# Batch transposes by DMA, a second buffer for values, a third chunk over two PSUM pairs and a new engine order in a sparse-attention and MLP kernel

## The reference

```python
scores = scale * np.matmul(q, k.transpose(0, 1, 3, 2))
mask_local = (rel >= 0) & (rel < stride)            # stride = 32, heads 0 to 3
mask_strided = (rel >= 0) & (pos[None, :] % stride == pos[:, None] % stride)   # heads 4 to 7
attn = softmax(where(mask, scores, -1e9)) ; attn_out = attn @ v
x = attn_out.transpose(0, 2, 1, 3).reshape(B * S, H * D)      # 4608 x 512
h = x @ w_in                                                  # 512 -> 2048
P = a[0] + a[1] * h + a[2] * h**2 + a[3] * h**3
Q = 1.0 + abs(b[0]) * abs(h) + abs(b[1]) * h**2
out = (P / (Q + 1e-6)) @ w_out                                # 2048 -> 512
```

## Time and profile before

| | us |
|---|---|
| median of 13 runs | 410.68 |
| lowest and highest of them | 408.20, 414.85 |
| the profiled execution | 408.66 |
| its span, first to last instruction | 406.5 |
| DVE busy | 328.6 |
| PE busy | 330.7 |
| ACT busy | 269.7 |

### The profile page before, as it was taken

One profiled execution on the slowest core, in us unless ns is written; L12 is line 12 of the kernel. 1 busy time (PEld: TensorE's weight loads), 2 busy tenths in 40 slices (PEclk: granted clock), 3 DMA queues, 4 the chain that ended last, 5 costly groups with the idle time before them and its releaser, 6 DMA issues.

```text
span 406.5 us, 9652 instructions
## 1 busy us (share of the span) xinstructions
PE 330.7 (81%) x4312; PEld 167.9 (41%) x4352; DVE 328.6 (81%) x279; ACT 269.7 (66%) x236; POOL 154.6 (38%) x203
## 2 busy tenths in 40 slices
PE   2499659988896998789998999997899889688530
PEld 2455334454453555335454544443344445343210
DVE  3539998999841148999999998899899799999930
ACT  3438938794864457985996896399279669685310
POOL 1968735935974992397074009300000000000000
PEclk9759958999999999969999999999699999999955
DMA  8999899879999997596295139443002201222002
GB/s 264 189 162 123 111 200 93 89 90 109 155 158 120 101 166 75 110 92 57 41 108 91 30 79 96 65 79 73 0 0 53 52 19 34 52 53 52 0 21 83
DMA packets 100121, 36.04 MB, mean 89 GB/s; under 512 B 71792, under 2 KB 95024, under 8 KB 100080
## 3 DMA queue, kind: packets, MB, share of 16 engines
q0 software_dynamic: 72800, 16.86, 46.7%
q1 hardware_dynamic: 27280, 18.57, 20.6%
HBM read 36.90 MB, written 9.44 MB: 114 GB/s over the span
## 4 chain that ended last, share of the span: by engine, by line
DVE 40%; PE 39%; ACT 8%; issue 6%; SPq 2%; DMA 2%; DVEq 0%
PE psH L578 16%; PE psO L578 13%; DVE UU L957 6%; DVE T L987 5%; DVE T L981 5%; DVE UU L954 4%; PE psS L578 4%; DVE T L977 4%; DVE T L942 3%; DVE T L984 3%; DVE T L974 3%; PE psA L578 3%; DVE T L979 3%; DVE XR L838 2%; ACT HB L928 2%
## 5 line engine op out<-in xcount | busy, mean ns | idle before, releaser
L578 PE MATMUL psO<-Wout,T 128*128 128x512 bf16 x473 | 113.9, 383 | 11.5 <-issue 3.7
L578 PE MATMUL psH<-XT,Win 128*128 128x512 bf16 x448 | 113.6, 398 | 9.4 <-ACT HB L928 8.9
L928 ACT ACTIVATE HB<-psH 128x1024 bf16<-128x1024 f32 x64 | 65.3, 1020 | 56.3 <-PE psH L578 56.1
L966 ACT ACTIVATE UU<-UU,cst 128x2048 bf16<-128x2048 bf16 (+1 forms) x38 | 72.5, 1909 | 11.9 <-DVE UU L957 11.9
L578 PEld LDWEIGHTS psO<-Wout,T 128*128 128x128 bf16 x512 | 47.5, 99 | 64.1 <-ACT OS L1051 4.8
L969 ACT ACTIVATE UU<-UU 128x2048 bf16<-128x2048 bf16 (+1 forms) x38 | 69.2, 1821 | 0.4
L578 PEld LDWEIGHTS psH<-XT,Win 128*128 128x128 bf16 x448 | 42.4, 99 | 65.1 <-ACT HB L928 12.2
L472 POOL DMA_DIRECT2D VL<-in_v_dram x28 | 24.5, 888 | 62.4 <-PE psA L578 62.0
L987 DVE TENSOR_TENSOR T<-T,UU 128x4096 bf16<-128x4096 bf16 (+2 forms) x23 | 41.6, 1824 | 3.2 <-ACT UU L969 2.8
L957 DVE TENSOR_TENSOR UU<-UU,T 128x4096 bf16<-128x4096 bf16 (+2 forms) x23 | 41.6, 1822 | 0.3
L977 DVE TENSOR_TENSOR T<-T,HB 128x8192 bf16<-128x8192 bf16 (+3 forms) x17 | 41.1, 2416 | 0.5
(11 more groups left out here) (137 smaller groups left out, 391.0 us busy)
## 6 DMA issues: line engine op xcount, KB each, us to landing
out_dram<-OS SPq DMA_DIRECT2D x72, 128.0 KB
kn<-in_k_dram POOLq DMA_DIRECT2D x14, 256.0 KB, 5.6
qn<-in_q_dram POOLq DMA_DIRECT2D x14, 256.0 KB, 6.1
Win<-in_moe_w_in_dram POOLq DMA_DIRECT2D x4, 512.0 KB, 9.8
Wout<-in_moe_w_out_dram POOLq DMA_DIRECT2D x1, 2048.0 KB, 15.6
VL<-in_v_dram POOLq DMA_DIRECT2D x28, 72.0 KB, 3.5
VT<-in_v_dram POOLq DMA_DIRECT2D x56, 32.0 KB, 2.9
VL<-VL SPq DMA_DIRECT2D x7, 153.0 KB, 3.1
```

Of the source, the lines that this page charges most:

```text
L578: return lambda e: e.matmul(out_ap, l, r, start=start, stop=stop, skip_group_check=True)
L928: o2 = add("ACT", (lambda a, hb=hb, ps=ps, f=f: a.activation(hb[:, f:f + 2, :], ps[:, :, :], AF.Copy)), [o1, old], ca(1024), key - 30)
L966: ln = add("ACT", (lambda a, u=u, zl=zl: a.activation(u[:, zl, :], u[:, zl, :], AF.Ln, bias=cst[:, 0:1], scale=1.0)), [d3, cons], 0.28 + w ...
```

## The change

- The strided heads' q and k of batches 1 to 7 are transposed by four DMA transposes per batch, issued by SP (step T), in place of R1 and the copy by DVE. Batch 0 keeps R1. `sT` has a new layout (head ahead of pair).
- The leftover rows of q and k of all batches are transposed by two DMA transposes per batch (step TL), in place of the 24 products and the copy to `LT` by ACT; a small copy by ACT into `kL` remains. The rows lie in `qm` and `km` in runs of 64 for that.
- The second batch's values get a buffer of their own inside `T3[2]`, idle until chunk 2 (`vi`); batch 2 then follows batch 0 in the ordinary buffer. The staging of batch 0's q and k moves to `HB[1]`.
- Chunk 2's steps alternate between pairs H and O as well (`NHO = 3`), and `dense2(c)` follows `dense1(c + 2)` in the program's order.
- `Wout` is loaded after R3 of batch 1; the values of batch 1 are issued ahead of the second half of `Win`; the identity is the first load of all.
- 70 matmuls of 128 columns on the identity (`fill`) depend on its load alone, have the highest keys and stand ahead of the last PE transpose of batch 0's attention.
- Nearly all keys come from a table by kind and by batch or chunk (`KT`, `Key`), so that the order on every engine is a new one.

```diff
+KT = {
+    "L": [-72.4, -237.8, -370.7, 323.1, 600.5, -236.5, -196.6, 245.0],
+    "S": [-680.0, 36.9, -286.2, -371.8, 156.5, 311.6, 229.2, 619.8],
+    "A": [-410.3, -115.4, 44.6, 115.1, -153.3, 41.1, -16.3, 133.2],
+    "AL": [-397.0, 199.6],
...
+    "XT": [-221.2, -555.1, -446.7, 242.3, -29.5, 235.2, 198.6, 337.0],
+    "HB": [95.1, 57.3, -165.0, -358.4, 31.9, -341.6, 222.2, 540.1, 102.5],
...
+class Key:
...
+    def of(self, kind):
+        return Key(kind, self.i, self.off)
+
+    def value(self):
+        return KT[self.kind][self.i] + self.off
...
-    SB, AB, MB, HL = 1.7, 0.0, 2.9, 4
+    HL, NHO, DA, TB, NF0 = 4, 3, 0, 1, 70
...
+    LT = A("LT", [128, 2, 4, 128], BF)
+    NV = 2
+
+    def vi(b):
+        return 1 if b == 1 else 0
...
+    VT = [A("VT0", [128, 4, 4, VS], BF)]
+    VW = [A("VW0", [128, 2, VS], BF)]
+    t3f = T3[2].rearrange("x f c -> x (f c)")
+    VL.append(t3f[:, 0:36 * VS].rearrange("x (m h d) -> x m h d", m=9, h=4))
+    VT.append(t3f[:, 36 * VS:52 * VS].rearrange("x (h g d) -> x h g d", h=4, g=4))
+    VW.append(t3f[:, 52 * VS:54 * VS].rearrange("x (j d) -> x j d", j=2))
...
-    c_idn = cload("c_idn", IDN, np.eye(128), -990)
+    c_idn = cload("c_idn", IDN, np.eye(128), -1005)
...
-    def load_wout(key):
+    def load_wout(key, dep):
         add("POOL", (lambda e: e.dma_start(Wout[:, :, :], w_out.rearrange("(f p) o -> p f o", p=128))),
-            [v_free[0]], 1.3, key, g2, 12.5)
+            dep, 1.3, key, g2, 12.5)
...
-    f32q = T3[2].rearrange("x f c -> x (f c)").bitcast(F32)
+    f32q = HB[1].rearrange("x f c -> x (f c)").bitcast(F32)
...
-        t3_free[2] = [ops]
+        hb_free[1] = [ops]
...
             load_v(1, -940, 0)
-            load_win(2, -930)
-            load_win(3, -929)
-            load_v(1, -920, 1)
+            load_v(1, -930, 1)
+            load_win(2, -920)
+            load_win(3, -919)
             for x in (1, 0):
                 load_qk(1, -909, 2, x)
             load_v(1, -908, 2)
-            load_wout(-890)
         else:
-            key = (b - 2.3) * P
+            key = Key("L", b)
+            if b == 2:
+                load_wout(key + 0.9, [n_free[0][1][0]])
...
+    fill = [add("PE", (lambda e: e.matmul(PS["H"][:, 1, 0:128], IDN[:, :], IDN[:, :], start=True, stop=True,
+                                          skip_group_check=True)), [c_idn], 0.1, 9000.0 + z) for z in range(NF0)]
...
-        base = (b - SB) * P if b > 1 else -100.0 if b else -300.0
+        base = Key("S", b)
...
-        order = ["R1", "R2", "R3", "S", "L", "X"]
+            sets.update(X="A")
+        order = ["T" if b >= TB else "R1", "R2", "R3", "S", "L", "TL", "X"]
         if first:
-            order = ["RL", "X"] if late else ["R1", "R2", "R3", "S", "L"]
+            order = ["TL", "X"] if late else ["T" if b >= TB else "R1", "R2", "R3", "S", "L"]
...
+            if name == "T":
+                tr = []
+                for x, T in ((1, K), (0, Q)):
+                    g = ch_t[x].group()
+                    for y in range(2):
+                        add("SP", (lambda e, x=x, T=T, y=y: e.dma_start_transpose(
+                            sT[:, x, 2 * y:2 * y + 2, :, :].rearrange("x h e p -> x (h e) p"),
+                            T[:, 4 + 2 * y:6 + 2 * y, :].rearrange("x h c -> x (h c)"))),
+                            [n_ev[x, 0, b], t_free["sT"]], 1.25, key.of("ST"), g, 0.6)
+                    n_free[x][0][i] = g.ops
+                    tr.append(g.ops)
+                evs["sT"] = tr
+            elif name == "TL":
+                g = ch_t[2].group()
+                for x, t in ((0, qm[i]), (1, km[i])):
+                    n_free[x][2][i] = g.ops
+                    add("SP", (lambda e, x=x, t=t: e.dma_start_transpose(LT[:, x, :, :], t[:, :])),
+                        [n_ev[x, 2, b], t_free["LT"]], 1.25, key.of("ST"), g, 0.6)
+                evs["LT"] = g.ops
+                evs["kLl"] = add("ACT", (lambda a: a.activation(
+                    kL[:, :, 544:608].rearrange("x a (p g) -> x g a p", g=4),
+                    LT[:, 1, :, 0:32].rearrange("x g (a p) -> x g a p", a=2), AF.Copy)),
+                    [g.ops, t_free["kLl"]], ca(128), key.of("XE" if first and name in ("TL", "X") else "SE"))
...
                 evs["kL"] = [e, ini[id(kL)]]
-            elif name in ("R3", "RL"):
...
-                    deps.append(n_ev[0, 1, b])
-                left = name == "RL" or not first
-                if left:
...
         v_free[iv] = avs
+        if iv == 1:
+            t3_free[2] = avs
...
-                pn = "HO"[npair[0] % 2] if c < 2 else "H"
+                pn = "HO"[npair[0] % 2] if c < NHO else "H"
...
-        if step >= 2:
-            dense2(step - 2, res[step - 2])
+        if step >= 3:
+            dense2(step - 3, res[step - 3])
```

More of the change, by code:

```diff
@@ L412, in bass_strided_sparse_attn__then__act_rational_pade_kernel @@
     ch_s = [chan(f"c_s{i}") for i in range(NV)]
+    ch_t = [chan(f"c_t{x}") for x in range(3)]
     ch_x = [chan(f"c_x{i}") for i in range(NX)]
@@ L650, in scores @@
                                              K[:, 2 * a + hh, 64 * g:64 * g + 64], IDN[:, :], True, True))
-                o1 = add("PE", makers, [n_ev[1, 1, b], c_idn, fr], 0.5 if b else 1.0, key)
+                o1 = add("PE", makers, [n_ev[1, 1, b], c_idn, fr], 1.0, key)
                 n_free[1][1][i] = [o1]
-                e = evac("ACT", kL[:, :, 32:544], ps[:, :, :], [o1, t_free["kL"]], key - 5, 1024)
+                e = evac("ACT", kL[:, :, 32:544], ps[:, :, :], [o1, t_free["kL"]], key.of("XE" if first and name in ("TL", "X") else "SE"), 1024)
@@ new lines, in scores @@
+                for a in range(2):
+                    for g in range(4):
+                        o = (a * 4 + g) * 128
+                        for hh in range(2):
+                            makers.append(tp(pb[64 * hh:64 * hh + 64, 0, o:o + 128],
+                                             Q[:, 2 * a + hh, 64 * g:64 * g + 64], IDN[:, :]))
+                o1 = add("PE", makers, [c_idn, fr, n_ev[0, 1, b]], 0.65, key)
+                n_free[0][1][i] = [o1]
+                e = evac("ACT" if b else "DVE", qL[:, :, :, :].rearrange("x a g p -> x (a g p)"), pb[:, 0, :],
+                         [o1, t_free["qL"]], key.of("XE" if first and name in ("TL", "X") else "SE"), 1024, True)
@@ L726, in scores @@
                                         "x g (r c) -> x c g r", c=2), False, False))
[L727 removed]
+                o1 = add("PE", makers, [evs["kL"], evs["qL"], c_mk, c_idn, fr], 0.85 if b else 1.5, key)
                 e = add("ACT", (lambda a, ps=ps: a.activation(EL[es][:, :, :], ps[:, :, :], AF.Exp, scale=0.125)),
[L729 removed]
+                        [o1, E_free[es]], ca(1024), key.of("XE" if first and name in ("TL", "X") else "SE"))
                 p_free[pn] = [e]
@@ L767, in scores @@
                     ps[:, :, 64:256].rearrange("x j (u i) -> x j u i", i=16), AF.Exp, scale=0.125)),
-                    [o1, E_free[es], ini[id(EW[es])]], ca(384), key - 5)
+                    [o1, E_free[es], ini[id(EW[es])]], ca(384), key.of("XE" if first and name in ("TL", "X") else "SE"))
                 p_free[pn] = [e1, e2]
@@ L856, in attend @@
                 ot = add("PE", [tp(pt[:, 128 * n_:128 * n_ + 128], x[:, 128 * n_:128 * n_ + 128], IDN[:, :])
-                                for n_ in range(4)], [o3, fr_, c_idn], 0.5 if b == 0 else 0.25, key + 0.4)
-                ev = evac("DVE" if T % 2 == 0 else "ACT", dst, pt.rearrange("x (n c) -> x n c", n=4), [ot, wait], key - 20, 512, True)
+                                for n_ in range(4)], [o3, fr_, c_idn, fill if b == 0 and T == 3 else []], 0.5 if b == 0 else 0.25, key + 0.4)
+                ev = evac("DVE" if T % 2 == 0 else "ACT", dst, pt.rearrange("x (n c) -> x n c", n=4), [ot, wait], key.of("N" if key.kind == "A" else "NL"), 512, True)
                 x_prev = fr_
@@ L889, in dense1 @@
     def dense1(c):
[L890 removed]
+        base = Key("M1", c)
         res = []
@@ L1058, in bass_strided_sparse_attn__then__act_rational_pade_kernel @@
     res = {}
-    for step in range(NCH + 2):
+    for step in range(NCH + 3):
         if step < B:
```

154 lines of the change are left out of this document (61 added, 93 removed), and 13 rows, old and new, of the table KT.

## The result

The changed kernel takes 404.61 us (median of 11 runs, 403.07 to 407.63) where the kernel before took 410.81 beside it; the ratio is 0.988, with a 95% interval of 0.985 to 0.991. The forecast was 373 us with a range of 357 to 396, so the sign came out as expected and the size did not. The profiled execution took 403.87 us, its span 401.8.

A forecast was written before the change was run, and what follows sets the result against it. VectorE was taken to bound the two long stretches, with a 28.7 us hole between; 26.1 (start) + 322.2 (work with pauses) + 3.0 (hole's rest) + 18.0 (end) = 369.3 us span, scaled to 373 us, range 357 to 396.

The forecast's parts named there:

- The work: VectorE's busy time from its first chunk step on: 315.4 us, less 8.5 for copies to `sT`, gives 306.9.
- the end: Eight matmuls, their copies and the stores after VectorE's last product: same code, so 18.0 us as before.
- The start: Before VectorE's first chunk step at 29.1 us: 3 us gained by fill and order (1 lost to 5 gained), leaving 26.1.
- the idle time: VectorE's pauses among its work: at a 95.2% share 306.9 us take 322.2, plus 3.0 for the hole's rest.
- three signs of being wrong: VectorE's idle time moves to a later chunk; TensorE waits for `sT` or `LT`; VectorE's first step isn't before 29.1 us.
- What takes their place: 44 more DMA transposes on SP: 5.0 to 10.9 us more latency per batch, 28 to 75 us of all engines, costed at nothing.
- The slow rival: First 150 us: SP's queue and DMA engines become the bound, late transposes costing up to 43.6 us; 417 us, chance 0.07.
- POOL's queue: Batch 1's values ahead of `Win`'s second half: `Win` issued up to 9 us later, costed at nothing, at worst 9 us.
- the rival of TensorE as the bound: From 29.1 us on, TensorE's work at an 88.5% ceiling sets the pace: 388 us; chance 0.22, shared with a half-open hole.
- The hole: VectorE's 28.7 us gap before chunk 2, from late values and TensorE's order: shrinks to 3 us, range 0 to 17.

The follow-up runs named there:

- tiny copies: The changed kernel with each of the 44 transposes by DMA replaced by a 16 x 32 copy on the same queue, same waits and order; 383.78 us.
- the run with narrow `dense2`: The run with tiny copies, with dense2's matmuls of chunks 0 to 7 cut from 512 to 128 columns, same order; 382.96 us.

## Why the prediction was wrong

In the prediction's own terms (profiled spans; the work is VectorE's busy time by chunk stretches, 40.93 + 35.30 + 38.68 + 33.31 + 160.50 in the changed kernel):

| term, us | forecast | changed | tiny copies |
|---|---|---|---|
| VectorE's first chunk step | 26.1 | 34.4 | 30.1 |
| its work from there on | 306.9 | 308.7 | 308.8 |
| its idle time among it | 18.3 | 41.5 | 25.1 |
| after its last product | 18.0 | 17.2 | 17.3 |
| span | 369.3 | 401.8 | 381.3 |

The stretches of the changed kernel, and below of the run with tiny copies, cut at the first steps of chunks 0 to 4 (window, length, busy us and instructions of PE, PEld, DVE, ACT, POOL, granted clock, DMA share, GB/s):

```profile
34.40:92.60 58.20, 31.62 (x648) 17.46 (x649) 40.93 (x52) 34.83 (x34) 33.95 (x43) 0.74 1.49 141
92.60:130.40 37.80, 35.27 (x601) 17.49 (x601) 35.30 (x41) 29.87 (x30) 27.74 (x32) 0.95 1.47 131
130.40:182.40 52.00, 42.69 (x624) 20.57 (x631) 38.68 (x30) 36.18 (x32) 35.07 (x39) 0.93 1.14 124
```

```profile
30.10:78.10 48.00, 30.67 (x702) 17.50 (x701) 41.04 (x53) 35.35 (x35) 40.40 (x52) 0.80 1.30 131
78.10:117.50 39.40, 35.02 (x603) 17.09 (x602) 35.21 (x41) 29.48 (x29) 28.07 (x33) 0.98 1.40 120
117.50:163.20 45.70, 43.70 (x632) 20.62 (x631) 38.67 (x30) 35.91 (x32) 33.56 (x39) 0.96 1.11 117
```

The work and the end were right. The work is 1.8 us over the forecast, SP shows the 76 transposes foretold, and VectorE's busy time, forecast at some 320 us, is 321.8. The start and the idle time were wrong, by 31.5 us of span, and the transposes make 20.5 of that. Two of the prediction's three signs of being wrong stand in the trace: scores wait for `sT` (9.8 and 5.5 us), and VectorE's first step isn't earlier than 29.1.

*What takes their place: the step that failed.* It gave the 44 transposes latency and DMA time, both from rows, and then cost both at nothing: the latency "since scores run ahead of their chunk", the DMA time because it was "spread over some 260". The sizes were near. Latency of 7.1 to 13.0 us per batch was expected, and batch 1's took 15.1 (first issue at 34.28, last landing at 49.35), batch 2's 16.2, both above the range; the DMA time was to be 28 to 75 us of all engines, and 16.4 x 44 / 16 = 45 came. The cover was what failed. The cover of a chunk's 34 us was taken from the steady state, but in the first four chunks scores feed attention that the next chunk waits for. And the share of 1.10 to 1.23, quoted for the slow rival, should have said that in that stretch the time of a transfer comes out of other transfers.

*The slow rival* had the place right (SP's queue and the DMA engines, before 180 us) and the mechanism by half. It priced latency alone, at up to 43.6 us, and gave it 0.07. Waiting for `sT` and `LT` on TensorE and ScalarE turned out to be 5.4 us; the other 15.4, what the transposes do to their queue and to other transfers, stood in none of its terms.

*The Trainium skill* (Advanced Engine Details and Errata, section X-Bar Transpose (TRN2)) holds transposes as fast as regular DMAs. The measurement decides here: twice the DMA time of a plain copy of the same size, and 19.0 us of the kernel's time between the two. The prediction sided with the dearer row, and then didn't use it.

*The start.* Forecast 3 us earlier than before, measured 5.3 later. ScalarE's wait for `LT` makes 4 of these (30.4 without that wait). Of the 3 us hoped for, nothing came: the first step began 1.7 us later than before (0.8 less without the fill) and took 3.59 again. The rule cited there (the Trainium skill, TensorE: Matmul & The Clock Gate, section Part 1: The HAM clock gate), that activity releases the clock, is not refuted by this. From 14.6 to 26.1 us TensorE was busy for 5.4 of 11.5 us, with only five of the fill's matmuls among it, and the first step found the granted clock at 0.50.

*POOL's queue.* The second half of `Win` was to be issued up to 9 us later; it is 11.1 later (22.98 to 34.09). The step costed this at nothing, for VectorE would be at other groups. But TensorE's order has batch 1's attention ahead of chunk 0's last group, and that waits for batch 1's values, which are loaded in the same stretch. In the run with tiny copies, TensorE and then VectorE:

```profile
45.06 0.30 PE L637 MATMUL psA<-T,EL 64*32 64x65 bf16 x8 [4.88 <-DMA T<-T]
```

```profile
58.22 0.21 DVE L885 RECIPROCAL RC<-psH 128x8 f32<-128x8 f32 x1 [5.16 <-PE psH L637]
```

Even that run misses the forecast span by 12.0 us: 4.0 at the start, 6.8 in VectorE's idle time and 1.9 in its work, less 0.7 at the end. The 5.16 us are the longest of its waits after the start. Next is the stretch to chunk 3, where VectorE idles for 7.0 of 45.7 us and TensorE is busy for 43.7. That is the rival of TensorE as the bound, held to one stretch: at most some 4 us by the run with narrow `dense2`.

*The hole.* Its rest was taken at 3, with chunk 2 near 105 us. It came at 130.4, at 117.5 without the transposes, and both the causes named were real (12 to 13 us each). What was missed is that the hole is a delay of everything up to chunk 2 and can open again before chunk 3: the forecast looked for the next thing late only inside the stretch of the hole.

## What to carry to other kernels

Price an operation that moves to the DMA engines in the stretch where it runs: where their share is already full, its time comes out of other transfers, however early its own result is. A cover taken from the steady state does not hold for the first chunks, where every queue is in order and nothing is ahead. And before a transpose goes to DMA for want of room on VectorE, time a plain copy of the same tiles in its place: the difference is the price of the turning.

## What the runs showed of the hardware

A transpose by DMA slows loads on the other queue: twelve loads of batch 1's values, which depend on no transpose, land in 7.2 and 12.3 us beside transposes, in 5.1 and 6.7 beside copies of the same bytes. A wait costs TensorE twice, since after the 9.81 us at 75.7 the granted clock is 0.50, the 1.2 GHz level, and chunk 1's next step takes 3.60 us in place of 1.90:

```profile
75.70:85.50 9.80, 0.00 (x0) 0.00 (x0) 7.24 (x5) 4.11 (x3) 0.38 (x1) 0.67 1.20 182
85.50:95.00 9.50, 6.76 (x144) 3.29 (x144) 5.35 (x6) 6.01 (x7) 2.40 (x4) 0.50 1.37 175
```

```profile
91.33 3.60 PE L634 MATMUL psH<-XT,Win 128*128 128x512 bf16 x8 [0.29 <-ACT HB L977]
```

And 24,576 more packets of a load, at 64 elements each, cost nothing that could be measured.
